# Attention with rotary embedding, then a two-layer projection: TensorE's attention written out without a loop, and the start of the second half moved

## The reference

```python
def _attn_ref(q, k, v):                        # each (4, 8, 576, 64), float32
    q_rot, k_rot = rotate(q), rotate(k)        # rotary embedding: cos and sin tables
    scores = 1 / sqrt(64) * q_rot @ k_rot.T
    attn = exp(scores - max(scores))
    return (attn / (sum(attn) + 1e-9)) @ v
def reference(...):
    x = attn_out.transpose(0, 2, 1, 3).reshape(2304, 512)
    h = x @ w_in                               # 512 x 2048
    g = max(h, 0) + alpha * min(h, 0)          # alpha: one number per column of h
    return g @ w_out                           # 2048 x 512
```

## Time and profile before

| | |
|---|---|
| median of 3 runs | 672.91 us (672.4 to 675.45) |
| the profiled execution | 672.58 us, of which the profile's span is 670.8 us |
| TensorE busy | 656.0 us, 98% of the span |
| VectorE, ScalarE, GpSimd busy | 338.8, 320.7, 266.8 us |
| attention, periods 0 to 16 | up to about 270 us |
| TensorE's mean granted clock | 0.997 of full speed |

### The profile page before, as it was taken

How to read it: one execution, slowest core, us unless ns; L and a number is a source line. 1 busy time by engine, 2 the same in 40 slices (tenths; PEclk the granted TensorE clock), 3 DMA queues, 4 the chain that set the end, 5 groups by cost and what they waited for, 6 DMA issues and landing times.

```text
span 670.8 us, 15166 instructions
## 1 busy us (share of the span) xinstructions
PE 656.0 (98%) x5570; PEld 561.7 (84%) x5570; DVE 338.8 (51%) x779; ACT 320.7 (48%) x730; POOL 266.8 (40%) x254
## 2 busy tenths in 40 slices
PE   8899999999999998999999999999999999999998
PEld 7677787777877776898899999999999999999996
DVE  4687777767888764445522332233233323332222
ACT  2788888868888875333332223222322232223223
POOL 3766788858865323222222222222222222222222
PEclk9999999989999999999999999999999999999999
DMA  6596554444554336000010001000100010001001
GB/s 148 153 229 178 124 136 110 106 105 103 120 121 104 83 117 251 1 1 1 1 48 0 1 1 47 1 1 0 47 0 0 0 47 0 0 0 48 1 0 48
DMA packets 73311, 41.62 MB, mean 62 GB/s; under 512 B 59812, under 2 KB 64292, under 8 KB 72740
## 3 DMA queue, kind: packets, MB, share of 16 engines
q1 hardware_dynamic: 72978, 40.62, 23.1%
q10 hardware_dynamic: 274, 0.16, 0.1%
HBM read 22.95 MB, written 4.72 MB: 41 GB/s over the span
## 4 chain that ended last, share of the span: by engine, by line
PE 94%; ACT 2%; DVE 1%; issue 1%; DMA 0%; SPq 0%; POOL 0%; ACTq 0%; DVEq 0%
PE banks L753 30%; PE banks L782 30%; PE banks L697 9%; PE banks L595 8%; PE banks L671 5%; PE banks L622 3%; PE banks L693 3%; PE banks L644 2%; PE banks L569 2%; PE banks L649 1%; ACT prob L824 1%; ACT pt L867 1%; DMA cos_sb<-in_cos 0%; PE banks L577 0%; PE banks L652 0%
## 5 line engine op out<-in xcount | busy, mean ns | idle before, releaser
L517 POOL TENSOR_TENSOR g_lo<-g,g_hi 128x384 fp32r<-128x384 f32 (+1 forms) x98 | 99.7, 1018 | 309.2 <-ACT g_hi L936 299.8
L1100 DVE TENSOR_SCALAR g<-banks,alpha_sb 128x384 f32<-128x384 f32 (+1 forms) x98 | 59.7, 610 | 250.9 <-ACT pos L927 250.9
L753 PE MATMUL banks<-x_hi,w_in_lo 128*128 128x384 f32 x384 | 129.3, 337 | 0.0
L753 PE MATMUL banks<-x_hi,w_in_hi 128*128 128x384 f32 x384 | 129.2, 337 | 0.0
L753 PE MATMUL banks<-x_lo,w_in_hi 128*128 128x384 f32 x384 | 129.0, 336 | 0.0
L927 ACT ACTIVATE pos<-banks 128x384 f32<-128x384 f32 x96 | 47.1, 491 | 170.2 <-PE banks L753 170.2
L782 PE MATMUL banks<-w_out_hi,g_hi 128*128 128x512 f32 x288 | 114.9, 399 | 0.3
L782 PE MATMUL banks<-w_out_hi,g_lo 128*128 128x512 f32 x288 | 112.9, 392 | 0.0
L782 PE MATMUL banks<-w_out_lo,g_hi 128*128 128x512 f32 x288 | 111.9, 388 | 0.0
L936 ACT ACTIVATE g_hi<-g 128x384 fp32r<-128x384 f32 (+1 forms) x98 | 50.9, 519 | 115.9 <-DVE g L1103 115.9
L824 ACT ACTIVATE prob<-prob,nmax 128x576 f32<-128x576 f32 x128 | 98.2, 773 | 1.3 <-DVE prob L991 1.2
(11 more groups left out here) (80 smaller groups left out, 917.3 us busy)
## 6 DMA issues: line engine op xcount, KB each, us to landing
q_swap<-q_nat SPq DMA_DIRECT2D x32, 256.0 KB, 3.7
k_swap<-k_nat SPq DMA_DIRECT2D x32, 144.0 KB, 3.1
out<-stage SPq DMA_DIRECT2D x18, 256.0 KB, 2.0
raw_q<-in_q SPq DMA_DIRECT2D x32, 128.0 KB, 2.9
raw_k<-in_k SPq DMA_DIRECT2D x32, 128.0 KB, 2.5
raw_v<-in_v SPq DMA_DIRECT2D x32, 128.0 KB, 2.3
w_in_raw<-in_moe_w_in SPq DMA_DIRECT2D x4, 1024.0 KB, 5.8
w_out_raw<-in_moe_w_out SPq DMA_DIRECT2D x8, 512.0 KB, 7.5
```

The lines of the kernel that those rows point to most:

```text
L517: nc.gpsimd.tensor_tensor(g_lo[f % 2][:, part], g[f % 2][:, part], g_hi[f % 2][:, part].bitcast(F32), ALU.subtract).then_inc(g_lo_done, 1)
L753: mm = nc.tensor.matmul(h_ps[f % 2], w[:, j, cols], xx[:, j, :], start=(step == 0), stop=(step == 3 * CT - 1))
L1100: nc.vector.tensor_scalar(g[f % 2][:, part], h_ps[f % 2][:, part], 0.0, alpha_sb[:, f:f + 1], ALU.min, ALU.mult).then_inc(neg_done, 1)
```

## The change

1. TensorE's attention: `batches(pe, batch)` becomes a Python loop, so the sixteen periods stand one behind the other in its program. The other engines keep their loops. The program of TensorE has 2422 merged rows, where it had 2246.
2. TensorE's period 16: `hidden(0, 0, 0)` moves from behind the first `pv` to behind the first small transposition (U_KQREM), `hidden(0, 0, 1)` from behind the second `pv` to between U_PB[0] and U_PB[2]. The first now waits for the maxima of period 15's eighth tile but not for its exponentials.
3. ScalarE and VectorE: the high and low parts of x for chunk 0 (4 operations on each) move from period 16 to period 15. The first `positive`, `high`, `high_w_out`, `gate` and `low_w_out` move forward within period 16.

```diff
+        def is_closing(p):
+            return isinstance(p, int) and p == PERIODS - 1
...
# TensorE, period
                 spread(p, t, U_KQREM)
+                if not has_now(p):
+                    hidden(0, 0, 0)
                 score(p, t, REM_TILE)
                 turn(p, t, U_QREM)
                 turn(p, t, U_KREM)
                 turn_two(p, t, U_PB[0])
+                if not has_now(p):
+                    hidden(0, 0, 1)
...
                 pv(b, t, 0)
-                if not has_now(p):
-                    hidden(0, 0, 0)
...
                 pv(b, t, 1)
-                if not has_now(p):
-                    hidden(0, 0, 1)
# TensorE, hidden
                     if f == 0:
-                        pe.wait_ge(exp_done, PERIODS * TILES - 1)
+                        pe.wait_ge(max_done, PERIODS * TILES - 1)
# TensorE, the attention
-            batches(pe, batch)
+            for b in range(NB):
+                batch(b)
             period(NB, 0)
# ScalarE, period
                 exps(p, t, REM_TILE)
+                if not has_now(p):
+                    positive(0, 0, 0)
                 flat(p, U_PB[2], t)
                 if not has_now(p):
+                    high_w_out(0)
+                    high(0, 0, 0)
+                if is_closing(p):
                     for j in range(CT):
                         high_x(j)
-                    high_w_out(0)
...
                 flat(p, U_INV, t)
-                if not has_now(p):
-                    positive(0, 0, 0)
-                    high(0, 0, 0)
# VectorE, period
                 flat(p, U_PB[3], t)
+                if not has_now(p):
+                    dve.wait_ge(alpha_in, 16)
+                    gate(0, 0, 0)
+                    low_w_out(0)
                 maxima(p, t, A_TILES[2])
...
+                if is_closing(p):
+                    for j in range(CT):
+                        split_x(0, 0, j)
...
-                if not has_now(p):
-                    for j in range(CT):
-                        split_x(0, 0, j)
...
                 normalise(p, *before, 0)
-                if not has_now(p):
-                    low_w_out(0)
-                    dve.wait_ge(alpha_in, 16)
-                    gate(0, 0, 0)
```

## The result

| | before | changed |
|---|---|---|
| median, in the comparison after the forecast | 673.65 us (672.4 to 675.45, 4 runs) | 667.42 us (667.3 to 667.66, 4 runs) |
| ratio | | 0.990 (95%: 0.987 to 0.993) |
| the profiled execution | 672.58 us, span 670.8 | 667.3 us, span 665.5 |

The forecast was 667.4. The sum behind it was not as good as that: two of its terms were too small, and a loss that it didn't have hid this. (The median of the kernel before has moved too, from the 672.91 us that the forecast started from, so the two medians lie 6.2 us apart, not 5.5.) That shows in the profile after. First its page: span, the strip of TensorE's granted clock, and the chain that ended last by engine, which answer to the earlier trace rows.

The account below looks back on a forecast made before the run. TensorE, busy 98% of the span, was taken as the bound, so only its idle or low-clock time could be won. -4.07 - 1.37 + 0.1 = -5.34 us gave 667.4 us, own range 666.6 to 668.4, whole range 666.2 to 669.6.

Parts of the forecast that it names:

- The gap and the low clock behind it: TensorE's attention loop, jump between periods 7 and 8: 2.58 us too long, then 1.49 at low clock; both go, -4.07 us.
- the other engines' jumps would take the gap's place: Rival, between periods 7 and 8: ScalarE, VectorE and GpSimd still jump, TensorE waits; 668.4 to 670.7 us, chance 0.12.
- Waits with constants for numbers in registers: TensorE's written-out periods: replacing register numbers in waits by constants was counted as no gain, from period 13's 14.83 us.
- Period 16, 1.37 us: TensorE's waits ahead of U_QREM (0.65) and U_PB's second half (0.72) vanish behind moved products; 0.78 ahead of U_MIXED stays.
- The x parts fit in period 15: Operations moved to period 15: ScalarE's cost nothing, VectorE's four subtractions cost 0 to 0.2 us, taken as 0.1.
- The collision with GpSimd's split: Rival, period 15: GpSimd starts splitting the last slab first and holds off VectorE's fourth subtraction; 1.1 us, 668.5, chance 0.12.
- The rival that the low clock shows up elsewhere: The gap goes, but the clock falls once at another place, such as period 16; 1.49 us, 668.9, chance 0.08.

## Why the prediction was right, and where it was not

- **The gap and the low clock behind it go with the loop.** Right: the loop put back brings both back (2.80 us and a period of 16.35), and writing out alone takes both away. That the other engines' jumps would take the gap's place was given 0.12; no wait of TensorE appears there. (which the prediction names for what ScalarE and VectorE waited for behind the gap, shows TensorE's rows alone.)
- **"Waits with constants for numbers in registers therefore give nothing that I count."** Wrong, and the step that failed. It was read from batch 3, whose period 13 takes as long as one in the loop. But its neighbours in the same trace, periods 12 and 14, are written out as well and were shorter. Their first rows:

```profile
196.19 0.28 PE L640 MATMUL banks<-ident,prob_rem 128*64 128x64 f32 x4
...
240.49 0.28 PE L640 MATMUL banks<-ident,prob_rem 128*64 128x64 f32 x4
```

  With the rows of period 13 and 14 in the earlier trace rows, period 12 took 210.92 - 196.19 = 14.73 us and period 14 took 240.49 - 225.75 = 14.74. In the changed kernel all such periods take about 14.73, and with a short loop 14.80 to 14.87 again. Why period 13 took 14.83 us with constants (14.88 with the moves alone, the other kernel that has the old loop) stays open. Periods 2 to 15 gave 5.3 us in the profile without low clock (211.75 to 206.45), where 4.07 were forecast. Against periods of 14.73 the gap and the low clock are 33.71 - 29.46 = 4.25 us. The other six periods of the loop, 4 to 6 and 9 to 11, gave 0.86, of which 0.37 are period 5's: it took 15.12 us. With the moves alone, the same loop had 14.83 there, so most of that is no cost of the loop. The last 0.2 lie in periods outside it.
- **Period 16, 1.37 us.** Mis-sized: 1.65 (15.48 to 13.83), with writing out alone 15.31 and with the moves alone 13.68, so 1.5 to 1.8 as one pairs them. The idle times in brackets end at a modelled end of the product before; the spacing of starts is what counts.
- **The x parts fit in period 15, 0.1 us.** Right: periods 15 with and without them, 251.44 - 236.78 = 14.66 and 253.09 - 238.48 = 14.61, are 0.05 apart. The collision with GpSimd's split (0.12) did not come; in this execution the order was not close, because the slab landed 2.8 us later against the rest.
- **The rival that the low clock shows up elsewhere** had 0.08 and the price of 1.49 us. It came true in the profile (1.87 us at the start), but the runs speak against an effect of the change: mean clocks of the kernel before go down to 0.987, where its profile has 0.997 with the loss behind the jump alone, and the kernel with the loop and the moves shows the low clock at the start. No profile shows the kernel before itself with it. The sum was made against an execution without this loss. That the median before was 672.95 to 674.8 in later comparisons fits this.

So -5.34 was forecast; the change itself is worth 5.3 + 1.65 = 6.95 us in TensorE's program between two executions without low clock at the start (spans 670.8 and 663.7, 7.1 apart), and in the changed kernel's first profile 1.87 of them were lost again. The mechanism was right, but that the time came within 0.1 us was luck: two terms too small met one left out.

## What to carry to other kernels

In this kernel the jump of a loop of two periods cost nothing that shows, and that of a loop of four cost 2.25 to 2.8 us and a fall of the clock worth 1.5 us more: look in the instruction queue whether the second pass loads code, and shorten or write out. The loop form itself took some 0.1 us a period where short products stand between the waits, and nothing that shows where long ones do. When one row of several like it is read as the price of something, look at its neighbours. Compare spacings of the same row in successive periods, not idle times, and look at the granted clock of every execution before a single profile is made the basis of a sum.

## What the runs showed of the hardware that was not expected

- Two executions of one program, with the same wait of 2.19 us at the same place, kept the clock in one and lost it for some 6.8 us in the other (period 2 began 1.9 us later). With 14 products of zeros in the wait the mean clock was 1.0 in all six executions of one kernel and in two of four of another, with 9 in four of six, with 6 in three of six. No profile with zeros, even only 6, has the fall behind that wait. In the profiles with 9 and 6 of them they end by the time the wait would, and the first transposes start no later.
- The loop of four periods was loaded anew in its second pass with 7 blocks, one of two periods with none at all in 120 us.
- The loop of two periods, with waits at registers' numbers, took 0.1 to 0.12 us a period more than the same periods written out.
